# Delta-rule attention, dense layer and top-1 experts on one core: routing done tile by tile through lists in memory, and one program part instead of two

## The reference

```python
# 1. delta rule, for each of 4 batches x 8 heads, 768 steps, head size 48
y[t] = q[t] @ state;  state += beta[t] * outer(k_n[t], v[t] - state.T @ k_n[t])
# x is y as 3072 tokens x 384
# 2. dense layer, 384 -> 2048 -> 384
h = np.maximum(x @ w_in, 0.0);  x1 = h * h @ w_out
# 3. experts: 8 of them, 384 -> 1024 -> 384, one for each token
logits = x1 @ w_gate;  expert = argmax(logits);  gate = softmax(logits)[expert]
out[token] = gate * (np.maximum(x1[token] @ w1[expert], 0.0) @ w2[expert])
```

## Time and profile before

| | us |
|---|---|
| median of three runs | 1084.79 (1083.94 to 1086.43) |
| the profiled execution, its own time | 1085.38 |
| its span, first to last instruction | 1083.8 |
| PE busy in the span | 908.6 (84%) |
| DVE busy | 481.0 (44%) |
| ACT busy | 417.9 (39%) |
| POOL busy | 186.8 (17%) |

### The profile page before, as it was taken

One profiled execution on the slowest core, in us unless ns is written; L12 is line 12 of the kernel. 1 busy time (PEld: TensorE's weight loads), 2 busy tenths in 40 slices (PEclk: granted clock), 3 DMA queues, 4 the chain that ended last, 5 costly groups with the idle time before them and its releaser, 6 DMA issues. The chain is left out here.

```text
span 1083.8 us, 25997 instructions
## 1 busy us (share of the span) xinstructions
PE 908.6 (84%) x10359; PEld 777.0 (72%) x10360; DVE 481.0 (44%) x951; ACT 417.9 (39%) x728; POOL 186.8 (17%) x119
## 2 busy tenths in 40 slices
PE   3254999999999999999999992469289999894995
PEld 3253788788788878888888872448279999793995
DVE  6988877457555734743112114933114442131220
ACT  4233556643753574364345441012123333221331
POOL 2000000000000000000000001457455450584011
PEclk9985999999999999999999995569789999896998
DMA  7016569537633944563385516635565351622000
GB/s 286 2 52 238 166 235 391 181 119 261 260 102 119 382 136 139 189 232 126 101 281 192 196 48 242 252 110 160 174 247 219 129 208 63 251 98 86 22 21 6
DMA packets 36604, 182.13 MB, mean 168 GB/s; under 512 B 4542, under 2 KB 7780, under 8 KB 30114
## 3 DMA queue, kind: packets, MB, share of 16 engines
q1 hardware_dynamic: 30242, 144.83, 37.1%
q0 software_dynamic: 6272, 35.99, 9.1%
HBM read 154.05 MB, written 28.12 MB: 168 GB/s over the span
## 5 line engine op out<-in xcount | busy, mean ns | idle before, releaser
L604 DVE TENSOR_TENSOR h_l<-h,h_h 128x512 fp32r<-128x512 f32 x96 | 66.3, 691 | 198.3 <-ACT h_h L359 198.3
L351 ACT ACTIVATE relu<-HP 128x512 f32<-128x512 f32 x96 | 57.4, 598 | 197.0 <-PE HP L875 196.8
L886 PE MATMUL ACC<-h_h,ring 128*128 128x512 f32 x288 | 117.0, 406 | 3.1 <-DVE h_l L604 3.1
L873 PE MATMUL HP<-x_h,ring 128*128 128x512 f32 x288 | 117.3, 407 | 1.6 <-DVE x_l L597 1.6
L1222 POOL TENSOR_TENSOR we_l<-raw_e,we_h 128x3072 fp32r<-128x3072 f32 x16 | 108.1, 6771 | 51.5 <-DMA we_h<-in_w 45.5
L874 PE MATMUL HP<-x_h,ring 128*128 128x512 f32 x288 | 113.4, 394 | 0.0
L875 PE MATMUL HP<-x_l,ring 128*128 128x512 f32 x288 | 113.2, 393 | 0.0
L1023 POOL MEMSET ones_sq<- 128x128 f32 x1 | 0.2, 204 | 654.4 <-POOLq L52 654.4
L887 PE MATMUL ACC<-h_h,ring 128*128 128x512 f32 x288 | 112.7, 391 | 0.0
L888 PE MATMUL ACC<-h_l,ring 128*128 128x512 f32 x288 | 112.4, 390 | 0.0
L1360 PE MATMUL EH<-we_h,xT_h 128*128 x186 | 78.5, 422 | 30.7 <-POOL we_l L1222 28.4
(11 more groups left out here) (191 smaller groups left out, 1736.5 us busy)
## 6 DMA issues: line engine op xcount, KB each, us to landing
ring<-w_scratch SPq DMA_DIRECT2D x80, 768.0 KB, 4.5
raw_e<-in_w SPq DMA_DIRECT2D x16, 1536.0 KB, 6.4
we_h<-in_w POOLq DMA_DIRECT2D x16, 1536.0 KB, 9.9
w_scratch<-ring SPq DMA_DIRECT2D x16, 768.0 KB, 4.4
kT<-in_kT SPq DMA_DIRECT2D x6, 1024.0 KB, 11.8
kk<-in_k SPq DMA_DIRECT2D x6, 1024.0 KB, 9.6
qT<-in_qT SPq DMA_DIRECT2D x6, 1024.0 KB, 11.1
vv<-in_v SPq DMA_DIRECT2D x6, 768.0 KB, 6.1
```

The lines of the kernel that those rows point to most:

```text
L873: pe.matmul(HP[n % 2][:, :], win_h[:, cols], x_h[:, k, :], start=k == 0, stop=False)
L886: pe.matmul(ACC[m][:, :], wout_h[:, cols], h_h[n % 2][:, :], start=f == 0, stop=False)
```

## The change

- The two parts become one: one set of programs, with expert SBUF tiles laid over those of the delta rule (`we_h`, `we_l`, `raw_e`) and of the dense layer (`rows` and the slot's tiles), and the same PSUM banks.
- Routing of tile t is done inside dense tile t+1, on 4 columns: DVE `choose` in block 6 and `gates` and `places` in block 8, ACT one Exp (`exponentials`) in block 6, PE `ranks` (eight float32 matmuls) in block 7.
- The place of a token is now in a region of its expert, 3072 places long, in a list in memory (`buckets`, pairs of token and gate, filled with an empty token at the start). POOL's `give_names` scatters the pairs, 4 indirect DMAs of 128 pairs for each tile. At the end one indirect DMA fetches 32 lines of 128 pairs (`names`), and PE turns them into `ids` and `gate_of`. `slots` on DVE finds which line is which slot.
- The weights of experts 0 and 1 are fetched and split during the last dense tiles: casting DMAs after the last rows of the delta rule have been stored, SP's loads in blocks 12 and 14 of tile 4 and 6 and 11 of tile 5, and the subtraction in 16 pieces of 768 columns. POOL does them between `give_names(3)` and `give_names(4)`.
- Last tile: all four logits first, then the turned rows into four other banks, then `ranks`.
- POOL's gathers: each of the first three has its own semaphore, and no weights stand between them. The scatters: one behind each expert's weights (slots 0 to 5), the rest after; after every fourth POOL waits until all have landed.
- SP: `store_x1` moves from block 7 to block 10; two stores that fill `buckets` come before the first `rows`.

```diff
+def give_names(t):                                   # POOL
+    after(pool, given[t % 2], 16 * B * (t // 2))
+    pool.iota(token[t % 2][:, :, 0:1], [[S, B], [0, 1]], base=C * t, channel_multiplier=1, **exact).then_inc(named, 1)
+    pool.wait_ge(named, t + 1)
+    pool.wait_ge(gate_done, t + 1)
+    pool.wait_ge(placed, t + 1)
+    for b in range(B):
+        pool.indirect_dma_start(out=buckets[:, :], out_offset=...place_i[t % 2][:, b:b + 1]...,
+                                in_=token[t % 2][:, b, :], ...).then_inc(given[t % 2], 16)
+def expert_lo(i):
+    e, n, c = i // 8, i // 4 % 2, i % 4
+    if c == 0:
+        pool.wait_ge(raw_in[n], 16 * e + 16)
+        pool.wait_ge(hi_in[e][n], 16)
+    cols = slice(W1 * n + PART * c, W1 * n + PART * (c + 1))
+    last = pool.tensor_tensor(we_l[:, e, cols], raw_e[:, cols], we_h[:, e, cols].bitcast(F32), ALU.subtract)
+    ...
+pool.wait_ge(blank_out, 32)
+for t in range(NCH - 2):
+    give_names(t)
+pool.wait_ge(y_out, 32 * NCH)
+for e in range(2):
+    for n, (w, part) in enumerate(halves):
+        pool.dma_start(we_h[:, e, part], w[e]).then_inc(hi_in[e][n], 16)
+for i in range(2 * WE // PART):
+    expert_lo(i)
+for t in range(NCH - 2, NCH):
+    give_names(t)
+...                                                  # both given[p], line_done
+pool.indirect_dma_start(out=names..., in_=buckets..., in_offset=...line_i[0:NS, :]...).then_inc(names_in, 16)
+pool.wait_ge(names_in, 16)
+pool.wait_ge(x1_out, 16 * (NCH + 1))
+def ranks(t):                                        # PE
+    pe.wait_ge(chosen_done, t + 1)
+    cols = chosen[:, :, :].rearrange("p b e -> p (b e)")
+    pe.matmul(RK, upper[:, :], cols, start=True, stop=False)
+    for b in range(1, B):
+        pe.matmul(RK[:, NE * b:], ones[:, :], cols[:, 0:NE * (B - b)], start=False, stop=False)
+    for b in range(B):
+        last = pe.matmul(ADD, ones[:, :], cols[:, NE * b:NE * (b + 1)], start=False, stop=b == B - 1)
+    last.then_inc(ranked, 1)
-for b in range(B):                                   # PE, last tile
-    turn(NCH - 1, b)
-    gate_logits(NCH - 1, b)
+for b in range(B):
+    gate_logits(NCH - 1, b)
+pe.wait_ge(relu_done, NF1 * NCH)
+for b in range(B):
+    for m in range(KD):
+        last = pe.transpose(turn_bank[b][:, 128 * m:128 * (m + 1)], x1T[:, m, C * b:C * (b + 1)], ident[:, :])
+    last.then_inc(last_turned, 1)
+ranks(NCH - 1)
+pe.wait_ge(names_in, 16)
+pe.wait_ge(placed, NCH)
+for o in range(2):
+    last = pe.transpose(AUX[:, NS * o:NS * (o + 1)], names[:, :, o], ident[0:NS, 0:NS])
+last.then_inc(names_turned, 1)
+def choose(t):                                       # DVE: six operations on 4 columns x 8 experts
+    ...
+def gates(t):                                        # DVE: waits for the Exp; sum, + eps, reciprocal
+    ...
+def places(t):                                       # DVE: waits for ranks; five operations
+    ...
+def slots():                                         # DVE, once: 16 small operations to line_i, 5 to control
+    ...
+    dve.wait_ge(names_turned, 1)
+    dve.tensor_copy(ids[:, :], AUX[:, 0:NSLOT]).then_inc(routed, 1)
+    then(dve.tensor_copy(gate_of[:, :], AUX[:, NS:NS + NSLOT]))
+    dve.sem_inc(routed, 1)
-weights_hi(0, 0)                                     # POOL, second part
-weights_hi(1, 1)
-weights_lo(0, 0, 0, 0)
-weights_lo(0, 0, 0, 1)
 pool.wait_ge(routed, 1)
-gather(0, FIRST)
-weights_lo(1, 0, 1, 0)
-gather(FIRST, GROUP - 1)
-weights_lo(1, 0, 1, 1)
-for first in range(GROUP - 1, NSLOT, GROUP):
-    gather(first, first + GROUP)
-with pool.Fori(0, NE // 2 - 1) as j:
-    weights(2 * j + 2, j + 1, 0)
-    weights(2 * j + 3, j + 1, 1)
-for s in range(NSLOT):
-    ...                                              # scatter slot s
+for s in range(FIRST):
+    gather(s, first_rows[s])
+for first in (FIRST, *range(GROUP - 1, NSLOT, GROUP)):
+    end = first + GROUP - first % GROUP - 1 if first == FIRST else first + GROUP
+    for s in range(first, end):
+        gather(s, gathered)
+    pool.wait_ge(gathered, 16 * (end - FIRST))
+for e in range(2, NE):
+    weights(e)
+    scatter(e - 2)
+for s in range(NE - 2, NSLOT):
+    scatter(s)                                       # if s % 4 == 3: pool.wait_ge(scattered, 16 * s + 16)
-...                                                  # routing over all 24 columns, one-hot tiles and PM
```

More of the change, by code:

```diff
@@ L30 @@
 GATE_EPS = 1e-9
+CAP = NT
+NPLACE = NE * CAP
+EMPTY = NPLACE // 128
+NS = 32
+WE = KD * F2 + NF2 * DM
+W1 = KD * F2
+PART = 768
 FIRST = 3
@@ new lines, in dense_tiles, with sb @@
+def dense_tiles(nc):
+    with ExitStack() as space:
+        def sb(name, shape, dt=F32):
+            return space.enter_context(nc.sbuf_tensor(name, shape, dt))
+        return dict(
+            ring=sb("ring", [128, NRING, 4, DM], F32R), x_raw=sb("x_raw", [128, KD, TILE]),
+            x_h=sb("x_h", [128, KD, TILE], F32R), x_l=sb("x_l", [128, KD, TILE], F32R),
+            relu=[sb(f"relu{p}", [128, TILE]) for p in range(2)], h2=[sb(f"h2{p}", [128, TILE]) for p in range(2)],
+            h_h=[sb(f"h_h{p}", [128, TILE], F32R) for p in range(2)],
+            h_l=[sb(f"h_l{p}", [128, TILE], F32R) for p in range(2)],
+            x1T=sb("x1T", [128, KD, TILE]), x1=sb("x1", [128, B, DM]), wg=sb("wg", [128, KD, NE]),
+            upper=sb("upper", [128, 128]), ones=sb("ones_sq", [128, 128]), back=sb("back", [128, NE]),
+            region=sb("region", [128, NE]), filled=[sb(f"filled{p}", [128, NE]) for p in range(2)],
+            lower=sb("lower", [128, NE, NE]), steps=sb("steps", [128, NCOL]), slot_no=sb("slot_no", [1, NSLOT]),
+            slot_p=sb("slot_p", [128, 1]), slot_q=sb("slot_q", [128, 1]),
+            token=[sb(f"token{p}", [128, B, 2]) for p in range(2)], line_i=sb("line_i", [128, 1], I32),
+            columns=[sb(n, [128, B]) for n in ("top", "total", "place")],
+            place_i=[sb(f"place_i{p}", [128, B], I32) for p in range(2)],
+            chosen=[sb(n, [128, B, NE]) for n in ("shifted", "expo", "chosen", "rank")])
@@ L57, in sem @@
             return ctx.enter_context(nc.semaphore(name))
[L59 to L96, removed]
@@ L120, in front @@
[L120 to L132, removed]
@@ L1407, in build @@
-def build(nc, kT, qT, k, v, beta, w_raw, w_gate, w1, w2, out):
-    ctx = ExitStack()
-    with ctx:
         w_scratch = nc.dram_tensor("w_scratch", (NF1, 128, 4, DM), F32).ap()
```

2322 lines of the change are left out of this document (1180 added, 1142 removed).

## The result

The changed kernel takes 1056.27 us in the median of 4 runs (1053.96 to 1057.76), the one before 1084.37 (1083.54 to 1086.43): ratio 0.9736, 95% interval 0.971 to 0.9762. The sign was right. The gain is 28 us where 58 were forecast, and the time lies 8 us above the top of the range. The profiled run took 1057.63 us (span 1055.4), 1.4 above the median.

The account below looks back on a forecast made before the run. PE bounds the dense tiles, a chain through all engines the stretch behind them, then POOL's queue. From 1085.4: -37.1 - 16.5 - 17 + 8 + 3 = -59.6, so 1026 us; range 1012 to 1048.

Parts of the forecast that it names:

- part b: First gather to slot 5: no half weights between POOL's gathers, 83.4 us becomes 66.9, gain 16.5 us.
- Rival 3: Slots 0 to 4 slow among gathers, PE sets slot 5, ranks cheaper: within 5 us of forecast; shares its 0.62.
- Part c: Expert part: result scatters at most four in a row end the 29.7 us iteration, gain 17 us.
- rival 1: Lost iteration not from ungrouped scatters, or fours as harmful: scatter gain only 0 to 5, 1038 to 1043 us; chance 0.17.
- Part a: Last x1T copy to first gather: 58.8 us becomes 21.7, gain 37.1 us.
- the landing 3.0: Behind the dense layer: the last list scatters land 3.0 us after issue, taken from the gathers' landing.
- Part d: Dense tiles: ranks costs PE 8 us over five tiles; small DVE terms, table loads and weight traffic cost little or nothing.
- the prediction's own signs: Dense tiles growing over 4 us refute Part d or Part e; PE gaps beside list scatters refute the forecast.
- Part e: Tiles 4 and 5: POOL's subtraction pieces may hold DVE's h_l, 1 to 5 us, or nothing.
- rival 2: Dense layer or lists dearer: piece trains hold h_l 21 us, or lists land 13 late; 1039 to 1047 us; chance 0.10.
- Rival 4: Dense tiles: each group of four list scatters costs PE 20.2 us, 101 in all; 1144 us; chance 0.04 for slower.
- Rival 5: POOL late with expert 1's weights, so give_names late; each us beyond 8 spare adds one, 1035 us; chance 0.06.

Follow-up runs that it names:

- the kernel with the three edits: Changed kernel with 64-byte pair rows, half weights of experts 0 and 1 issued one at a time, weights of experts 2 and 3 between the gathers; 1029.50 us.
- the best kernel: The kernel with the three edits, but 32-byte pair rows, x1 store in block 14, and POOL's first subtraction waiting for the last tile's x_l; 1023.85 us.
- the combined kernel: The kernel with the three edits, here with pairs in rows of 32 bytes instead of 64; 1027.95 us against 1029.50.

## Why the prediction was right or wrong

- **What bounds the kernel, and part b:** right. -16.7 against -16.5, with the wait for `we_l` before slot 5 where it was said. PE waits 9.60 us there, where 10 was said. Taking it away gave 12.8, since the slots among the gathers were quicker too. Rival 3 falls.
- **Part c:** right. 15.2 of 17 us came and no iteration is over 14.0 us but the one before slot 5. The grouping alone explains it (19.4 on the kernel before); rival 1 falls. The missing 1.8 stand at the end: from the issue of the last scatter to the end of the span it is 11.0 us where it was 8.9. One argument against rival 1 was misread: "none of the other iterations loses over 2.1". One near 931 took 14.1 us before, with 4.34 of waiting for `we_l`; it is 14.0 after, so nothing hangs on it.
- **Part a:** -30.0 for -37.1. Every step stood within a microsecond but one: "the landing 3.0". The wait in which it lies was 10.40, so the gathers were the wrong row for a scatter of neighbouring 8-byte pairs. The bounds named there, 5 us less and 13 more, held it; the value taken was 7.4 too low.
- **Part d is the step that failed.** `ranks` (2.0 us of PE busy, 2.3 us in tile 2) and the table loads (five of 1.28 us, for which no wait of PE shows) were right. Wrong were its last sentence, the weights "on top of 175 and 142 GB/s over some 100 us, with the ring four blocks ahead: nothing, 5 at most", and what the sum didn't contain at all, a price for what the list scatters do to other DMAs. I priced bytes over 100 us, and what counts is what stands in front of the ring for 35 us: four halves were asked for at once, beside the raw loads. Measured: 8.7 us for the burst; some 8.5 us for the lists in the tiles, or 11 to 13 with their landing at the end. Two of the prediction's own signs of this came: tiles 1, 3, 4 and 5 grew by over 4 us, and PE shows a gap beside list scatters.
- **Part e:** the holding was right, its price in this kernel too high. In the kernel after, h_l is held to 1.64 us at most, and PE waits 0.6 us for it in tiles 4 and 5, where 1 to 5 were said. In the kernel with the three edits the ring is no longer late, the x_l of the last tile meet the subtraction, and they lose 4.3 us. By the Trainium skill, "SBUF — State Buffer", section "Who interferes with whom", a two-input DVE instruction contends with a GpSimd instruction that reads SBUF. These traces agree, with 6.15 and 5.16 against 1.90 us. I had weighed the rule and looked for its victim in h_l alone.
- **The rivals:** what came is nearest to rival 2 (lists later, dense tiles dearer), but 9 us over its upper end and with another mechanism than it named: no train of pieces held h_l to its end. Rival 4 (lists stall PE at each group) had the right place and a price far off: some 8.5 us in all where it had 101, 5.2 of it in tile 1. It had been argued away by the gathers, which carry 1.5 KB a row. Rival 5 falls: POOL was ready for the last lists and stood 10.25 us until their places were there.

The sum of what was missed: 21.1 us more in the tiles, 1.4 ahead of them, 7.1 in a, 1.8 in c, less 0.2 in b are 31.2. The spans give the same, 59.6 - 28.5 = 31.1. The two causes found account for some 17 of the 22.5 us in and ahead of the tiles. Of the rest, up to 3.5 lie ahead of tile 1, where traces differ by as much.

**Open.** In the best kernel the last x1T still ends 17.8 us later than in the kernel before (666.8 against 649.0), where 11 was forecast. The largest piece is tile 1 (102.7 against 97.3 + 2.3), where PE stands about 2 us on "issue" and then runs at 1.2 GHz for a while, even without list scatters. Packets of the instruction queue come later there in all changed kernels (the first after 277.3 us before, 278.7 to 288.0 in them), behind 25 to 30 us of full DMA engines. That the two belong together is argued, not shown; what would make the fetch come earlier wasn't tried. Nor is it settled why neighbouring 8-byte rows are slow. The edits with wider rows also spread the list over four or eight times the memory and changed how the blanks are written and where the names are fetched to. Only leaving the scatters out and doubling them, with rows as before, point to the scatters by themselves.

## What to carry to other kernels

A DMA term is not its bytes over a long window: ask what is queued in front of the load that the bound engine needs next, and issue bulk loads one at a time where PE lives on a ring. Price scatters of a few bytes to neighbouring rows by what they do to the other DMAs, and space the rows: 64 bytes apart they cost 11 to 13 us less here, and whole rows of 32 bytes did as well in the combined kernel. When a two-input DVE operation and a GpSimd subtraction are near each other, look at every DVE operation of the stage, since removing one delay moves the collision to another.

## What the runs showed of the hardware

- Behind four indirect scatters of 128 rows of 8 bytes side by side (4 x 1 KB) the 16 DMA engines are busy for about 15 us and move only 87 to 200 GB/s. The time is in the packets of the other loads and stores (100.2% of 16 engines' time), not in the scatters' own (0.4%). With the rows at a distance of 64 bytes, the same 8 bytes leave 400 GB/s, and the wait for them falls from 10.40 to 5.35 us. The Trainium skill, "DMA: Bandwidth & Descriptors", section "Why small descriptors are slow (HBM only)", names costs per packet; they would be the same in both, so by them alone no difference would show. The measurement decides.
- A second set of such scatters costs again: 18.3 us by the medians. PE's longest gap in tile 1 is 2.5, 7.0 and 11.5 us for none (in tiles 0 to 3), one and two sets.
- PE stood idle for 7.0 us and came back at the 1.2 GHz level (granted clock 0.50 from 290 to 295), so a gap costs more than its length: tile 1 lost 7.8 us beyond `ranks` for a gap of 7.0.
- 22 scatters of rows of 1.5 KB without a pause cost 19.4 us; in fours with a landing between them, nothing that can be seen (the slots stay at 9.5 us).
